# Attention's row projection as two row tiles woven into the transposes

## The reference

```python
# attention: batch 4, 8 heads, 576 positions, head size 64
scores = scale * q @ k.T
thresh = max(scores, -1) - tau
scores = where(scores >= thresh, scores, -1e9)
attn = softmax(scores)                  # sum + 1e-9 in the denominator
x = (attn @ v), heads side by side      # 2304 tokens x 512
# experts: 8, hidden 1024
logits = x @ w_gate + modality_bias[modality_id]
e_idx, gate_w = argmax, its softmax probability
x = gate_w * (relu(x @ w1[e_idx]) @ w2[e_idx])
# second block, hidden 2048
h = x @ w_in
out = (h * tanh(softplus(h))) @ w_out
```

## Time and profile before

| | us |
|---|---|
| median of three runs | 951.83 |
| lowest and highest | 951.74, 952.17 |
| the profiled execution | 950.58 |
| its span, first to last instruction | 948.9 |
| TensorE busy | 919.1 |
| VectorE busy | 675.5 |
| ScalarE busy | 509.0 |

### The profile page before, as it was taken

The page is one execution under the profiler, slowest core; times in us unless marked ns, Lnnn a source line. Parts: engine busy times, 40 slices in busy tenths (PEclk is TensorE's granted clock), DMA queues, the critical chain, the costliest instruction groups (busy, mean ns, idle before and its releaser), DMA issues.

```text
span 948.9 us, 19389 instructions
## 1 busy us (share of the span) xinstructions
PE 919.1 (97%) x6976; PEld 771.2 (81%) x6977; DVE 675.5 (71%) x1227; ACT 509.0 (54%) x987; POOL 476.6 (50%) x560
## 2 busy tenths in 40 slices
PE   6999998999999999999999989999999999999996
PEld 4777776777778788888878878889898889899985
DVE  7999998999966411111152898878888788788793
ACT  5777777778752422222254564545545455555552
POOL 5222244657332654000000586786777777776884
PEclk9999999999999999999999999999999999999999
DMA  4131346232124573111225100100001000000000
GB/s 130 55 100 51 102 140 239 97 108 85 42 83 169 143 272 92 46 37 47 80 86 218 45 1 1 35 34 19 24 27 35 33 2 0 34 1 1 34 1 34
DMA packets 21937, 65.97 MB, mean 70 GB/s; under 512 B 3552, under 2 KB 3552, under 8 KB 21600
## 3 DMA queue, kind: packets, MB, share of 16 engines
q1 hardware_dynamic: 14512, 39.90, 12.3%
q0 software_dynamic: 4896, 20.00, 6.2%
q10 hardware_dynamic: 2448, 5.01, 1.9%
HBM read 46.63 MB, written 18.27 MB: 68 GB/s over the span
## 4 chain that ended last, share of the span: by engine, by line
PE 61%; DVE 4%; issue 4%; ACT 1%; ACTq 1%; POOL 0%; POOLq 0%; DVEq 0%
PE psum L1417 6%; PE psum L1419 6%; PE psum L1418 6%; PE psum L1409 6%; PE psum L1407 6%; PE psum L1408 6%; PE psum L1080 3%; PE psum L1082 3%; PE psum L1081 3%; PE psum L1107 3%; PE psum L1109 3%; PE psum L1108 3%; DVE rr L1529 2%; PE psum L1091 2%; PE psum L1066 1%
## 5 line engine op out<-in xcount | busy, mean ns | idle before, releaser
L1529 DVE RECIPROCAL rr<-rr 128x384 f32<-128x384 f32 x96 | 244.1, 2543 | 10.0 <-ACT rr L1477 10.0
L1355 POOL TENSOR_TENSOR uu<-uu,ex 128x384 f32<-128x384 f32 x96 | 97.2, 1013 | 100.9 <-ACT uu L1471 100.8
L577 ACT ACTIVATE prob<-ssb,smin 128x576 f32<-128x576 f32 x144 | 111.6, 776 | 66.5 <-DVE ssb L699 66.3
L1407 PE MATMUL psum<-x2T_hi,w_in_hi 128*128 128x384 f32 x384 | 131.0, 341 | 4.3 <-DVE gg L1535 2.7
L1409 PE MATMUL psum<-x2T_hi,w_in_lo 128*128 128x384 f32 x384 | 129.6, 338 | 0.0
L1408 PE MATMUL psum<-x2T_lo,w_in_hi 128*128 128x384 f32 x384 | 129.1, 336 | 0.0
L1161 DVE TENSOR_TENSOR hT_lo<-psum,hT_hi 128x512 fp32r<-128x512 f32 x38 | 26.3, 691 | 140.6 <-ACT hT_hi L1138 135.5
L699 DVE TENSOR_SCALAR_CACHE_REDUCE ssb<-psum,tauk 128x576 f32<-128x576 f32 x144 | 112.1, 812 | 12.7 <-PE psum L422 11.0
L339 POOL TENSOR_TENSOR limit<-smin,margin 128x2 f32<-128x2 f32 (+1 forms) x80 | 57.4, 718 | 120.4 <-DVE ssb L699 119.8
L1417 PE MATMUL psum<-w_hi,g_hi 128*128 128x512 f32 x288 | 114.5, 397 | 0.0
L1477 ACT ACTIVATE rr<-uu 128x384 f32<-128x384 f32 x96 | 50.5, 526 | 118.6 <-POOL uu L1355 118.6
(11 more groups left out here) (210 smaller groups left out, 2126.5 us busy)
## 6 DMA issues: line engine op xcount, KB each, us to landing
qk<-in_qk_dram SPq DMA_DIRECT2D x15, 640.0 KB, 3.9
vsb<-in_v_dram SPq DMA_DIRECT2D x16, 512.0 KB, 3.5
xrow<-xs ACTq DMA_DIRECT2D x17, 288.0 KB, 2.9
ys<-ysb SPq DMA_DIRECT2D x19, 257.0 KB, 3.0
stage<-in_w_in_dram POOLq DMA_DIRECT2D x16, 256.0 KB, 4.0
wa<-in_wa_dram SPq DMA_DIRECT2D x8, 512.0 KB, 7.0
wb<-in_wb_dram SPq DMA_DIRECT2D x8, 512.0 KB, 10.7
xs<-zrow SPq DMA_DIRECT2D x11, 288.0 KB, 2.8
```

The costliest lines, as they stand in the source:

```text
L577: act.activation(prob[:, n % 3, cols], ssb[:, w, cols], ACT.Exp, bias=smin[:, w, h:h + 1], scale=-1.0).then_inc(exp_done, 1)
L1407: pe.matmul(bank_of(n), w_in_hi[:, k, cols], xT_hi[w][:, k], start=(k == 0), stop=False)
L1529: dve.reciprocal(rr[:, n % 4], rr[:, n % 4]).then_inc(r_done, 1)
```

## The change

The projection of the rows becomes two row tiles: each head contracts over its own 64 partitions, takes its own 72 columns of `wx`, and writes all 128 tokens (`half_rows`). The near half (`rows_near`) is issued ahead of the transposes of the same step, the far half (`rows_far`) in their middle. Both halves write one PSUM bank, so the far half waits for a semaphore of the near half, `near_rows`. The transposes are started one block out of step (far block 1 with near block 0), and far block 0, which goes to the other bank, comes behind the far half of the rows. All turns are by row tiles now, that of tt = 1 too. The moved sums take one matmul over the far 64 partitions in place of two. The stand-alone calls of `rows_out` behind the loop run both halves one behind the other. `ranks` is issued ahead of the rows, with waits of its own.

```diff
-        def rows_out(n):
+        def half_rows(n, h):
             p, tt = divmod(n, TT)
-            c = (tt % 2) * 2 * HW
-            for h in range(2):
-                rows = slice(h * D, h * D + D)
-                last = pe.matmul(row_bank[rows, c:c + 2 * HW], otsb[:, n % 2, rows],
-                                 wx[:, p % HP].rearrange("p h c -> p (h c)"), start=True, stop=True)
+            c, rows = (tt % 2) * 2 * HW + h * HW, slice(h * D, h * D + D)
+            return pe.matmul(row_bank[:, c:c + HW], otsb[rows, n % 2], wx[rows, p % HP, h], start=True, stop=True)
+        def rows_near(n):
...
+                pe.wait_ge(rows_done, n)
+            half_rows(n, 0).then_inc(near_rows, 1)
+        def rows_far(n):
+            pe.wait_ge(near_rows, n + 1)
+            last = half_rows(n, 1)
             if tt == QT:
                 pe.wait_ge(summed, norms(n + 1))
-                for h in range(2):
-                    rows = slice(h * D, h * D + D)
-                    last = pe.matmul(moved[rows], t["shift"][:, rows], rsum[:, p % 2, 2 * QT:TPP], start=True, stop=True)
+                last = pe.matmul(moved, t["shift"][D:P], rsum[D:P, p % 2, 2 * QT:TPP], start=True, stop=True)
             last.then_inc(rows_done, 1)
+        def rows_out(n):
+            rows_near(n)
+            rows_far(n)
...
-        def turn(n):
+        def turn(n, rows_of=None):
...
+            if rows_of is not None:
+                rows_near(rows_of)
             pe.wait_ge(prob_done, units(n) + 1)
...
+            for b in range(3):
+                far(b + 1)
+                near(b)
+            if full:
+                pe.wait_ge(prob_done, units(n + 1))
+                far(QT)
+                near(QT - 1)
+            if rows_of is not None:
+                rows_far(rows_of)
+            if full:
+                half_block(rest_bank[:, D:2 * D], 1, 0).then_inc(far_turned, 1)
+                near(QT)
+                for b in range(QT + 1, blocks):
+                    far(b)
+                    near(b)
+                far(blocks)
+                pe.wait_ge(far_turned, halved(n))
+                half_block(rest_bank[:, 0:D], 0, blocks).then_inc(turned, 1)
+            else:
+                far(0)
+                near(QT - 1)
...
         for c in range(NS):
             scores(c)
             if c >= 4:
                 pv(c - 4)
-            if c >= 5:
-                rows_out(c - 5)
...
             if c >= 2:
-                turn(c - 2)
+                turn(c - 2, c - 5 if c >= 5 else None)
```

More of the change, by code:

```diff
@@ L183, in attention_phase @@
     far_turned = sem("far_turned")
+    near_rows = sem("near_rows")
     main_out = sem("main_out")
@@ L206, in attention_phase @@
     FAR = S
-    def by_half(n):
-        return n % TT != 1
     def halved(n):
-        return 3 * (n // TT) + n % TT + 1 - (n % TT > 0)
+        return QT * (n // TT) + n % TT + 1
     def both_halves(w, first, cols, apart):
@@ L221, in turned_block @@
     def turned_block(n, b):
[L223 to L226, removed]
+        return both_halves(n % 2, b * D, D, FAR)
     rank_bank, moved = psum[:, 7, 0:(TT + 1) * E], psum[:, 7, (TT + 1) * E:(TT + 1) * E + 1]
@@ L434, in turn @@
                 pe.wait_ge(main_out, n)
-            if n >= 1:
                 pe.wait_ge(rest_out, n)
             blocks = QT if not full else 2 * QT
-            if by_half(n):
-                def half_block(place, h, b):
-                    rows = slice(h * D, h * D + D)
[L442 to L470, removed]
+            def half_block(place, h, b):
+                rows = slice(h * D, h * D + D)
+                key = b * P if b < QT else (S + REM + (b - QT) * P if b < 2 * QT else QT * P)
+                return pe.transpose(place, prob[rows, w, key:key + P], ident[rows, rows])
@@ new lines, in near, with far @@
+            def near(b):
+                return half_block(turn_bank[:, 0, b * D:b * D + D], 0, b)
+            def far(b):
+                at = min(b, blocks) - full
+                return half_block(turn_bank[:, 1, at * D:at * D + D], 1, b)
+            for b in range(3):
[7 more added lines that the diff above has]
+                rows_far(rows_of)
@@ new lines, in turn @@
+            if full:
[10 more added lines that the diff above has]
+                near(QT - 1)
+                half_block(turn_bank[:, 1, QT * D:QT * D + D], 1, 2 * QT)
+                half_block(turn_bank[:, 0, QT * D:QT * D + D], 0, 2 * QT).then_inc(turned, 1)
@@ L516, in rows_out @@
                 pe.wait_ge(ranks_read, b + 1)
[L517 to L521 removed]
+            half_rows(n, 0).then_inc(near_rows, 1)
+        def rows_far(n):
+            p, tt = divmod(n, TT)
+            pe.wait_ge(near_rows, n + 1)
+            last = half_rows(n, 1)
             if tt == QT:
                 pe.wait_ge(summed, norms(n + 1))
[L524 to L526 removed]
+                last = pe.matmul(moved, t["shift"][D:P], rsum[D:P, p % 2, 2 * QT:TPP], start=True, stop=True)
             last.then_inc(rows_done, 1)
+        def rows_out(n):
+            rows_near(n)
+            rows_far(n)
         def ranks(b):
@@ L538, in tensor @@
                 pv(c - 4)
-            if c >= 5:
-                rows_out(c - 5)
             b, k = divmod(c - ROUTE, PER)
             if b >= 0 and k == RANK:
+                pe.wait_ge(rest_out, c - 2)
+                pe.wait_ge(x_done, norms(c - 5))
+                pe.wait_ge(rows_done, c - 5)
                 ranks(b)
             if c >= 2:
-                turn(c - 2)
+                turn(c - 2, c - 5 if c >= 5 else None)
         turn_x, up_half, down = early["pe"](pe)
@@ L584, in evacuate @@
                 act.wait_ge(pv_done, n - 1)
[L585 to L588, removed]
+            if n % TT < QT:
                 act.copy(pt[:, w, QT * P:QT * P + P], rest_bank).then_inc(rest_out, 1)
```

## The result

| us | before | after |
|---|---|---|
| median of four runs | 951.79 | 963.10 |
| lowest and highest | 951.71, 952.17 | 962.41, 964.17 |
| the profiled execution, its span | 950.58, 948.9 | 964.17, 962.5 |

The changed kernel is slower: 1.0119 times the kernel before, 95% interval 1.0102 to 1.0137, or +11.3 us. The direction was forecast, the size was not: 955.7 was predicted, and 963.1 lies above the range of 951 to 959. The two profiled executions are 13.6 us apart; the one of after is the slowest of its four, so the trace shows a little more than the median.

The account below looks back on a forecast made before the run. TensorE was taken to pace 131 us of attention, VectorE or a transfer the rest. Pairs +2.2, end of attention +2.0, scatter -0.3 made +3.9 us: 954.5 for the profiled execution, 955.7 as median; range 951.0 to 959.0.

Parts of the forecast that it names:

- Rival (a): Both halves' waits are hidden and the change is not slower: 949.5 to 953 us, best guess 951.2; chance 0.26.
- Rival (b): Each wait in the steps and tail costs the upper bound, 0.17 us: 959.5 us; chance 0.09.
- Rival (c): Row tiles do not overlap, so the four half passes come on top, 0.12 us more a step: 956 us; chance 0.05.
- each head's 72 columns are two passes on one row tile, a slot of 0.06 each: In the rows of a step, each half's two passes take 0.06 us each, as 144 columns stream in 0.12.
- Ordinary step: Step with eighteen transposes: 1.07 us for 0.96 from rows to next scores, waits included, 0.11 us lost.
- with the sums: The step with the moved sums, once a pair: an ordinary step's loss and 0.06 us more, +0.17 us.
- short turn: The step with ten transposes: 0.80 us for 0.70, 0.10 us lost.
- full width: The step with the full-width turn: 1.17 us for 1.39, 0.22 us gained by row tiles.
- The tail: Five stand-alone rows at the end of attention: 0.58 us for 0.24 each, with tiling switches +2.0 us in all.
- 8.2 pairs paced by TensorE: Pairs of heads in the 131 us that TensorE paces, at 15.94 us each; +0.27 a pair makes +2.2 us.
- in the order of the program: Matmuls of both tiles start in program order, so the weave hides half of the rows at best; 0.08 us gained without waits.
- 0.32 us at most: Where TensorE sets the pace, VectorE's idle time lets a pair shrink by only 0.92 - 0.60 = 0.32 us.

Follow-up runs that it names:

- experiment 4: The changed kernel with the far half of the rows directly behind the near half, ahead of all transposes; 982.63 us, ratio 1.0321.
- experiment 5: The changed kernel with the far half and far block 0 first, the near half only ahead of the near tile's last transpose; 956.34 us, ratio 1.0052.
- experiment 1: The changed kernel with the near half of the rows issued twice; 980.33 us, ratio 1.0305.
- Experiments 2 and 3: The changed kernel with one more matmul ahead of each near half, same weights, 8 or 144 moving columns; 981.73 us (ratio 1.0321) and 982.96 us (1.0346).
- experiment 8: The kernel before with only its full-width turn (tt = 1) by row tiles; 950.71 us, ratio 0.9999.
- experiments 9 and 10: The kernel of experiment 8 with eight transposes more in the turn of tile 1, or of tile 2; 952.22 us (ratio 0.9998) and 956.65 us (1.0037).
- 12: The kernel of experiment 8 with the scores of tile 1 moved into the middle of the turn ahead of them; 950.73 us, ratio 0.9984.

## Why the prediction was wrong in size

**What held.** The sign, and its mechanism: two halves in one bank have to be ordered, and the order costs more than the rows' shorter stream gives. The switch of tiling moved ahead of the rows, as forecast: from the last PV's group to the rows it was 222.45 - 222.23 = 0.22 us and is 221.32 - 221.01 = 0.31, 0.09 more for 0.10 forecast (the line of before is below).

```profile
222.23 0.39 PE L490 MATMUL psum<-pt,vsb 128*64 128x128 f32 x4
```

Rival (a), waits hidden, is refuted by the wait that stands open in experiment 4 and by the 0.97 us that experiment 5 gave back. Rival (b), 0.17 for a signal and the load behind it, is refuted by the timeline, where the two take 0.06 behind the modelled end of the half. That the time came out above even its 959.5 has another reason, the passes (and 959.5 already lay above the range that was to take it in). Rival (c), tiles that don't overlap, is refuted by the timeline: far transposes start at 221.33, between the near half's two passes.

**The step that failed: "each head's 72 columns are two passes on one row tile, a slot of 0.06 each".** A pass is 0.11 (experiment 1). Follow one ordinary step from its first pass to the near tile's next scores:

| us | forecast | trace of after |
|---|---|---|
| near half, first to second pass | 0.12 | 0.17 |
| second pass to the far half (end, signal, load) | 0.34 | 0.33 |
| far half, two passes, to far block 0 | 0.12 | 0.28 |
| far block 0 to the last transpose (far_turned) | 0.33 | 0.27 |
| last transpose to the scores | 0.06 | 0.12 |
| sum | 0.97 | 1.17 |

(In the trace 0.17 = 221.49 - 221.32 and 0.33 = 221.82 - 221.49; far block 0 starts at 222.10 and the last transpose at 222.37 inside the group at 222.01.) The two waits together were 0.60 for 0.67 forecast; the passes 0.45 for 0.24. The first wait came out right by luck: the pass in it lasts 0.27 where I had 0.23, the signal and the load take 0.06 where I had 0.11. So a step is 0.11 + 0.20 = 0.31 longer by this chain and 0.27 by the starts of its scores. All passes lie on one serial chain, near half, signal, far half, far block 0, signal, last transpose, so each pass's excess counts in full, in every step. I had taken the slot from the transposes of the earlier trace rows and from the stream of 144 columns, and both were the wrong row: before, the rows load 64 weight columns a pass in column tiles (137 ns), and the change turns that into 128 (184 ns). The 144 columns of before paced those passes (0.12 each) and hid their loads; with the stream halved and the loads doubled, the load is the longer of the two. Experiments 2 and 3 show that the stream does not set the price; that the load does rests on the starts of the loads, 0.11 apart, and on L502. The nearest row was in the trace and I did not read it: the scores' loads, 128 columns in fp32 on a row tile, take 187 ns.

The Trainium skill (TensorE: Matmul & The Clock Gate, LDWEIGHTS (loading the stationary operand)) says that a load takes P / 1.2 ns, P the weight's columns, however few rows are contracted; that makes 107 ns for 128 columns and 53 for 64, both estimates from the page's formula. The runs here agree with it for fp32 matmuls, 0.11 us a pass with 128 columns and 0.06 with 64 (L502); they don't for the transposes of the earlier trace rows, whose loads are also of 128 columns and which take 0.06 a pair. The prediction weighed the page on tiling and not this one. By its rule halving the contraction saves nothing on a load, and the change doubles the columns of each, so that a pass can't fall from 0.12 to 0.06.

**The signs that I named.** The second half comes 0.50 us behind the first (0.4 or more: right). The period is 17.22, not 16.2, and a stand-alone call 0.87, not 0.55 to 0.6: wrong, both by the passes. For the way from the first pass to the next scores I named 1.05 to 1.1 and the trace has 1.08 to the far tile's, but that sign was off against my own sum: its 1.07 held the switch, which lies ahead of the first pass, so 0.97 was what it meant.

**The terms.** Ordinary step +0.11 forecast, +0.27 measured; with the sums +0.17, +0.50 (their matmul stands on the same chain; its two passes add 0.23 where I had 0.06); short turn +0.10, about +0.25; full width -0.22, -0.01, which is the same 0.2 us missed. Sum of a pair +0.27, +1.28. The tail: +2.0 forecast, 3.4 by the trace; 0.87 us a call for 0.58, again four passes on one chain.

**The count.** 8.2 pairs paced by TensorE at +1.28 make 10.5 us; the loop gave 9.4. The sizes are close by luck, as the starts of the short scores in both traces show. Of the fifteen periods before only four lie within 0.05 us of 15.94; these grew by 1.24 to 1.29, together 5.1 us. Eight others grew by 0.2 to 1.1, together 6.2: "In the pairs that VectorE paces I count nothing" failed, since with steps this long TensorE holds those up too. Two hardly changed, and the one with the wait behind the scatter fell from 20.20 to 17.22, 3.0 where I had 0.3. The remaining 1.4 lie ahead of the first short scores (15.73 and 17.09 us). These last two vary from trace to trace: the kernel of experiment 8 has 18.24 for that pair and 17.06 for that start, with an ordinary period of 15.94 as before.

**That "the matmuls of both tiles" start "in the order of the program"** is false (221.33 stands before 221.49). It did not save the step, since the chain, not the shared order, set its length.

**That a pair can shrink by "0.32 us at most", by VectorE's idle time,** did not lead to the gain that I took from it. Experiment 8 took time from one step and won nothing; experiments 9 and 10 show that one step counts and another does not, and 12 won 0.3 us a pair over experiment 8 without making TensorE's work any shorter.

## What to carry to other kernels

Ask of every re-tiling how many weight columns a pass loads, before asking how many columns it streams: for the short fp32 matmuls of this case the load is the price, and splitting the contraction in two does not halve it. Two matmuls that must be ordered because they share a bank form a chain with all that waits behind them; put the two as far apart as the step allows, early and late: here that gave back 0.97 of 1.28 us a pair. And an engine that is 99% busy need not pace the loop in every step: adding a known piece of work to one step at a time shows which ones do.

## What the runs showed of the hardware

- An fp32 pass with 128 weight columns costs 0.11 us on its row tile, with 8 and with 72 moving columns, and 0.12 with 144 (periods 18.34, 18.35, 18.44 us for 17.22). With 64 weight and 64 moving columns on a column tile it costs 0.06 (L502).
- Row tiles run apart: the far tile's transposes start before matmuls of the near tile that stand ahead of them in the program. But an instruction that waits for a signal stops both (66 stalls, 13.7 us, in experiment 4).
- TensorE's signal to itself is short: from the end of the near half's last pass (221.49 + 0.27) to the start of the far half (221.82) it is 0.06 us, its load included; the end is the profile's modelled one, and from start to start it is 0.33. I had 0.11.
